# Turning probabilities on TensorE for two more steps, moving row sums, router roots and one key load in a fused attention and mixture kernel

## The reference

```
k_p, v_p = k.reshape(B,H,72,8,64).mean(3), v.reshape(B,H,72,8,64).mean(3)
attn = softmax(q @ k_p.T / sqrt(64));  x = (attn @ v_p) as 4608 x 512
h = x @ w_in;  g = max(h,0) + alpha*min(h,0);  x = g @ w_out          # 512 -> 2048 -> 512
logits = (x/|x|) @ (emb/|emb|).T / tau;  e = argmax;  gate = softmax(logits)[e]
out[token] = gate * (max(x[token] @ w1[e], 0) @ w2[e])                # 512 -> 1024 -> 512
```

## Time and profile before

| what | value |
|---|---|
| median of the runs | 1460.33 us |
| profiled execution, own time | 1461.15 us |
| its span | 1458.8 us |
| PE busy | 1403.1 us (96%) |
| DVE / ACT / POOL busy | 54% / 48% / 47% |
| mean granted clock of TensorE | 0.986 |

### The profile page before, as it was taken

One profiled execution on the slowest core, in us unless ns is written; L12 is line 12 of the kernel. 1 busy time (PEld: TensorE's weight loads), 2 busy tenths in 40 slices (PEclk: granted clock), 3 DMA queues, 4 the chain that ended last, 5 costly groups with the idle time before them and its releaser, 6 DMA issues.

```text
span 1458.8 us, 21254 instructions
## 1 busy us (share of the span) xinstructions
PE 1403.1 (96%) x7245; PEld 1152.0 (79%) x7245; DVE 792.8 (54%) x1498; ACT 693.1 (48%) x1022; POOL 687.7 (47%) x613
## 2 busy tenths in 40 slices
PE   8999989989989989989999999999999999999997
PEld 7887877868868767868788788888888878887876
DVE  7665766666757757757657576690002710066560
ACT  5434533433443443442433322544667666666664
POOL 4542243253243343342232233366666866577773
PEclk9999999999999999999999999999999999999999
DMA  8535242251352242332232220344433964369551
GB/s 249 173 108 153 67 120 67 60 125 56 75 119 60 68 114 59 82 91 70 47 87 52 59 87 22 135 167 130 96 88 80 219 185 98 79 145 238 143 113 26
DMA packets 204614, 153.57 MB, mean 105 GB/s; under 512 B 147036, under 2 KB 163420, under 8 KB 204384
## 3 DMA queue, kind: packets, MB, share of 16 engines
q1 hardware_dynamic: 59200, 99.20, 21.7%
q10 hardware_dynamic: 137280, 34.10, 14.4%
q0 software_dynamic: 8032, 18.93, 4.0%
HBM read 92.34 MB, written 29.43 MB: 83 GB/s over the span
## 4 chain that ended last, share of the span: by engine, by line
PE 72%; DMA 9%; DVE 6%; POOL 4%; issue 4%; ACT 3%; SPq 1%; ACTq 1%; DVEq 0%; POOLq 0%
PE y_ps L869 19%; PE h_ps L853 18%; PE y_ps L1010 14%; PE y_ps L976 14%; PE h_ps L813 2%; DMA shared<-in_k 2%; PE step_ps L769 2%; DMA x_dram<-shared 2%; DMA shared<-shared 2%; PE h_ps L988 1%; DMA shared<-in_v 1%; DVE weight_parts L1298 1%; POOL shared L1840 1%; DVE junk L1184 1%; POOL g_lo L1851 1%
## 5 line engine op out<-in xcount | busy, mean ns | idle before, releaser
L1851 POOL TENSOR_TENSOR g_lo<-g_full,g_hi 128x512 fp32r<-128x512 f32 x144 | 192.8, 1339 | 541.7 <-ACT g_hi L1536 541.7
L853 PE MATMUL h_ps<-x_hi_in,weight_parts 128*128 128x512 f32 x1144 | 373.5, 390 | 0.0
L869 PE MATMUL y_ps<-weight_parts,g_hi 128*128 128x512 f32 x1152 | 368.1, 401 | 2.1 <-POOL g_lo L1851 2.1
L869 PEld LDWEIGHTS y_ps<-weight_parts,g_hi 128*128 128x128 f32 x1152 | 218.4, 193 | 49.6 <-issue 2.4
L853 PEld LDWEIGHTS h_ps<-x_hi_in,weight_parts 128*128 128x128 f32 x1144 | 214.9, 188 | 44.6
L976 PE MATMUL y_ps<-weight_parts,x_hi_in 128*128 (+1 forms) x1032 | 242.0, 390 | 1.9 <-DVE weight_parts L1298 1.9
L869 PE MATMUL y_ps<-weight_parts,g_lo 128*128 128x512 f32 x576 | 228.5, 397 | 0.0
L976 PEld LDWEIGHTS y_ps<-weight_parts,x_hi_in 128*128 128x128 f32 x1032 | 193.3, 188 | 42.6 <-issue 2.7
L853 PE MATMUL h_ps<-x_lo_in,weight_parts 128*128 128x512 f32 x572 | 222.6, 389 | 0.0
L1165 DVE TENSOR_SCALAR g_full<-h_ps,alpha 128x512 f32<-128x512 f32 x144 | 107.7, 748 | 209.6 <-PE h_ps L853 207.4
L1536 ACT ACTIVATE g_hi<-g_full 128x512 fp32r<-128x512 f32 x144 | 90.7, 630 | 253.2 <-PE y_ps L869 171.0
(11 more groups left out here) (233 smaller groups left out, 1799.4 us busy)
## 6 DMA issues: line engine op xcount, KB each, us to landing
shared<-in_w SPq DMA_DIRECT2D x8, 2048.0 KB, 9.6
emb_all<-in_w SPq DMA_DIRECT2D x8, 2048.0 KB, 9.4
y_dram<-y_rows SPq DMA_DIRECT2D x9, 1024.0 KB, 4.4
shared<-in_q SPq DMA_DIRECT2D x34, 256.0 KB, 2.9
shared<-in_v SPq DMA_DIRECT2D x29, 288.0 KB
x_dram<-shared SPq DMA_DIRECT2D x32, 256.0 KB, 3.3
y_rows<-x_dram SPq DMA_DIRECT2D x32, 256.0 KB, 3.5
shared<-in_k SPq DMA_DIRECT2D x26, 288.0 KB, 3.7
```

Source lines behind the costliest of these rows:

```text
L853: mm = pe.matmul(h_ps[:, f % 2, :], w[:, k, f * P:(f + 1) * P], x[:, k, :], start=(n == 0), stop=(n == 3 * DC - 1))
L869: mm = pe.matmul(y_ps[:, j, :], a[:, f % 2, j * P:(j + 1) * P], w[:, f, :], start=(f == 0 and n == 0), stop=(f == FC - 1 and n == 2))
L1851: pool.tensor_tensor(gl[:, f % 2, :], g_full[:, f % 2, :], gh[:, f % 2, :].bitcast(F32), ALU.subtract).then_inc(gl_done, 1)
```

## The change

It has five parts. `TURN` becomes 10, so that steps 8 and 9 are turned by PE and the DMA turns from step 10 on. From step 10 on `row_scale` moves from the chunk behind the scores into the scores' own chunk (behind the first of the three dots, at chunk 12 behind `router_logits`), and `norm` with it, ahead of that chunk's `g_lo` on POOL. ACT's `root` moves from chunk 11 to chunk 9. SP issues the keys of chunk 12 ahead of the next tile's x, and DVE pools the keys of chunk 13 behind `router_choose` and `router_gate`.

```diff
-TURN = 2 * FIRST
+TURN = 2 * FIRST + QBUFS
@@ sync, tile
                         store_x(s)
+                        if 1 <= i <= BATCH - 3 and f in (6, 9, 12):
+                            load_k(PAIRS * (i + 2) + (f - 6) // 3)
                         if s == last_step(i + 1):
                             load_x(i + 1)
...
-                    elif i <= BATCH - 3:
-                        if f in (6, 9, 12):
-                            load_k(PAIRS * (i + 2) + (f - 6) // 3)
-                        elif f == FC - 1:
-                            sp.wait_ge(plane_joined, 2 * (last_step(i + 1) + 2 - TURN))
-                            load_k(PAIRS * (i + 2) + PAIRS - 1)
+                    elif i <= BATCH - 3 and f == FC - 1:
+                        sp.wait_ge(plane_joined, 2 * (last_step(i + 1) + 2 - TURN))
+                        load_k(PAIRS * (i + 2) + PAIRS - 1)
@@ vector, tile
                     s = sum_step(i, f)
-                    if s is not None:
+                    if s is not None and s < TURN:
                         row_scale(s)
...
-                        dots(i - 1, 3 * (f - 1), min(3 * f, DOTS))
+                        n = 3 * (f - 1)
+                        dots(i - 1, n, n + 1)
+                        if s is not None and s >= TURN:
+                            row_scale(s)
+                        dots(i - 1, n + 1, min(n + 3, DOTS))
...
-                    if n is not None:
+                    if n is not None and (i == 0 or f < 13):
                         sum_keys(n)
...
                         router_logits(i - 1)
+                        if s is not None and s >= TURN:
+                            row_scale(s)
                     if i and f == 13:
                         router_choose(i - 1)
                         router_gate(i - 1)
+                        if k_at(i, f) is not None:
+                            sum_keys(k_at(i, f))
@@ scalar, tile: root
-                    if i and f == 11:
+                    if i and f == 9:
@@ gpsimd, tile
                     s = sum_step(i, f)
-                    if s is not None:
+                    if s is not None and s < TURN:
+                        norm(s)
+                    s = score_step(i, f)
+                    if s is not None and s >= TURN:
                         norm(s)
```

## The result

The changed kernel took 1429.31 us (median of 4 runs, 1427.89 to 1430.99) against 1462.88 us of the kernel before on the same chip (4 runs): ratio 0.9772, 95% interval 0.9744 to 0.9800. Forecast were 1421 us and a range of 1413 to 1434. The direction and the main mechanism held; the gain was 33.6 us and not 39.5, and what is missing comes from waits at the ends of tiles, which I had priced at 1.0 us and which cost 9.5.

The account below looks back on a forecast made before the run. PE was taken to bound the kernel, leaving idle and low-clock time to win. Terms -22.1 - 9.4 - 7.9 - 1.4 - 1.6 + 1.9 + 1.0 = -39.5 gave 1421 us, range 1413 to 1434.

Parts of the forecast that it names:

- What bounds the kernel: Whole kernel: PE, busy 1403.1 of 1458.8 us; to win are 55.7 us of idle time and the low-clock time.
- Part 1: Chunk 13, tiles 1 to 5: keys asked earlier, pooled behind the choice; `ranks` waits go, -22.1 us, low clock behind, -9.4.
- Part 2: Chunks 6, 9, 12: sums and scaling one chunk up, roots at chunk 9; `values` waits -7.9 us, low clock at 621.6 -1.4.
- the floor of 1.5 us: Joins at chunks 6 and 9: 0.1 to 0.2 us of wait left at each of 10 places, 1.5 us of 9.4.
- The rule of the Trainium skill: DVE and POOL share an exclusive port pair: `norm` waiting for one dot cuts the 2.0 us gain to 1.4, two dots 0.8.
- Part 3: Steps 8 and 9 turned by PE: +1.9 us of turns, -1.6 us as the wait at tile 0's end goes.
- Part 4: Ends of tiles 1 to 5, without the turning pause: slow planes make `g_lo` of chunk 15 late, +1.0 us taken.
- A plane's way took up to 5.4 us: Ends of tiles 1 to 5: time from a plane's issue to the next copy, at most 5.4 us, used to time `g_lo`.
- the upper bound that I had given: Ends of tiles 1 to 5: with the slowest planes seen, 1.9 us late in each of five, 9.5 us.
- The rival of the tile ends: Tile ends: slow planes make a new wait, 3.9 us plus 1.9 of low clock in five tiles; 1449 us, chance 0.07.
- One of my own signs of being wrong: PE waiting for `g_lo` or next x at tile ends, or for joins at chunks 6, 9, 12 by over 0.5 us each.

Follow-up runs that it names:

- the two halves: Kernel before with one key edit each: keys of chunk 13 only pooled behind choice and gate, 1437.7 us; keys only asked for ahead of x, 1431.5 us.
- the turn back at step 8: Changed kernel with the DMA turning steps 8 and 9 again, sums and scaling still moved from step 10 on: 1427.7 us, ratio 0.9745.
- sums late: Changed kernel with row sums and scaling one chunk behind the scores again; keys, roots and turn as changed: 1433.0 us, ratio 0.9776.
- the root at 11: Changed kernel with the router's roots back at chunk 11, all else kept: 1425.1 us, ratio 0.9752.
- small x: Changed kernel with the x loads of tiles 2 to 6 fetching only 32 of 512 columns of each piece: 1415.8 us (one run).
- half of x later: Changed kernel with the third and fourth x piece of tiles 2 to 6 asked for behind the values' load of chunk 12: 1415.9 us, ratio 0.9649.
- after: The changed kernel itself, with all five parts, in its first profile, against the kernel before: 1429.31 us, ratio 0.9772.
- the keys alone asked ahead: Kernel before with one edit, SP asking for the keys ahead of x, DVE still pooling them ahead of the choice: 1431.5 us, ratio 0.9784.
- the change again: Changed kernel run once more, unaltered, on the same chip as later follow-ups: 1426.0 us, ratio 0.9762 to the kernel before.
- the values held: Changed kernel with the load of chunk 13's values held back at the ends of tiles 1 to 5 until x's last piece landed: 1437.1 us, ratio 0.9825.
- their pooling behind `g_lo`: Changed kernel with POOL's pooling of chunk 13's values moved behind `g_lo` of chunk 14: 1430.5 us, ratio 0.9762.

## Why the prediction was right, and where its size was off

**What bounds the kernel.** Right: each wait removed for good was won, and with the `ranks` waits the low clock behind them.

**Part 1 (-22.1 and -9.4).** Right, both. No `ranks` wait and no low clock at this place is left. I had counted the two halves as one edit; each alone does it. The low clock was counted too low: I had followed it for twelve matmuls, but it lasted longer. In the 6 us behind the waits of tiles 1 to 5 the clock of before was 0.65, 0.53, 0.74, 0.62 and 0.72, which loses 6 x 1.74 = 10.4 us, as in tile 2:

```profile
324.51:330.51 6.00, 6.00 (x20) 4.76 (x21) 3.52 (x15) 1.64 (x2) 0.39 (x1) 0.53 0.64 96
```

**Part 2 (-7.9 and -1.4).** Right as a step: all 9.4 us at `values` went, and the floor of 1.5 us that I had left at chunks 6 and 9 is not there. The root's move is worth the 6.2 us at chunk 12 and the sums' move the 3.1 us at chunks 6 and 9. The 6 us behind the wait of 621.64 ran at 0.72, so they lost 1.7 us and not 1.4. The rule of the Trainium skill (SBUF — State Buffer, Who interferes with whom) that spoke against the move was seen, and no wait at `values` came of it. A dot took a mean of 757 ns before and takes 849 now, and `norm` went from 1150 to 1361 ns, while the sums' second instruction went from 698 to 214:

```profile
L1183 DVE CUSTOM_DVE_ANT_0 junk<-y_rows,emb_all 128x512 bf16<-128x512 f32 x256 | 206.2, 849 | 0.3 <-issue 0.3
...
L1847 POOL TENSOR_TENSOR shared<-shared,row_scale 128x576 f32<-128x576 f32 x35 | 47.7, 1361 | 153.5 <-DVE row_scale L1142 153.5
```

These rows agree with the rule as I used it for the dots: in tile 2 a dot that began at 288.55, beside `norm` (288.09 to 289.63), took 1.63 us. The sums' second instruction reads a single tensor, so the two inputs that I named can't be what held it.

**Part 3 (+1.9 and -1.6).** Right within the noise: the whole 1.8 us at tile 0 went, and with the turn back at step 8 the time is the same.

**Part 4 (+1.0) is the step that was mis-sized.** "A plane's way took up to 5.4 us" was read from planes that left 3.7 us or more behind x. My working had the plane leave at 212.4, 3.0 us behind x, and kept that duration. It left only 0.7 us behind x in all five tiles and took 8.3 to 9.0 us. In tiles 2 to 5 the store's landing released it, the same that x waits for, as here in tile 2, where x was issued at 308.78:

```profile
308.77 0.69 ACT L1506 ACTIVATE shared<-shared 128x576 uint16<-128x576 uint16 x1 [2.02 <-DMA x_dram<-shared]
```

Even at the place that I had given it, planes took up to 7.3 us (sums late). And I had no term for the values of chunk 13, for which POOL stood 7.29 us in tile 1. The wait that followed was for `g_lo` of chunk 14, not of chunk 15 as I had followed it.

Measured: the `g_lo` line rose from 2.1 to 7.8 us, though the 1.8 us at tile 0 had gone. So the ends of tiles 1 to 5 cost 2.68 + 1.62 + 1.45 + 0.42 + 1.38 = 7.55 us of standing and, in tile 1 alone, 7.36 - 5.44 (two layers of 2.72) = 1.9 us of low clock: 9.5 us where I had 1.0. That this equals the upper bound that I had given is chance: that bound was five waits of 1.9 us for `g_lo` of chunk 15, with no low clock. The rival of the tile ends was right in kind and too high in price, since the low clock followed one wait out of five. One of my own signs of being wrong, a wait for `g_lo` at tile ends, did show.

**The sum with the measured terms.** -22.1 - 10.4 - 9.4 - 1.7 - 1.8 + 1.9 + 9.5 = -34.0, and the dense stage won 33.9. So the forecast missed part 4 by 8.5 us, and other terms that I had set too low (low clock, values, tile 0) gave 3.0 back. That the time still lay in the range owes something to this.

**Where the gain of part 2 went.** The root's move wins 6.2 us at chunk 12, and the tiles' ends take them back, as the run with the root at 11 shows by its equal time. The small x (1415.8 us) shows that x's transfer is the price, and half of x later (1415.9 us) shows that most of it can be had. Two engines stand at a tile's end. When the plane leaves early, POOL stands for the values (after); when it leaves late, ACT comes late to `g_hi` (sums late). Still open: why a plane that leaves 3.3 us behind x took 7.3 us with the sums late, while one 4.5 us behind took 3.5 us with the keys alone asked ahead; and in which part of the chip plane and x meet, for which no run was made.

## What to carry to other kernels

A duration of a transfer read from a trace belongs to the moment in which it ran: when an edit moves a transfer, look what is in flight at the new place, and price it with that company. Issuing it earlier can leave its end where it was. When two engines wait for two colliding transfers, reordering one engine's work only shows the other; split or delay the transfer that nobody needs soon. And a wait removed early in a repeated block counts only once the block's end has been followed to the next engine that stands.

## What the runs showed of the hardware

- A DMA transpose within SBUF (a plane) was back in 3.2 to 4.9 us when the x issued 0.7 us ahead of it was small, and took 6.2 to 10.6 us when that x was four loads of 256 KB (planes 0.7 us behind x in the change, the change again, the roots at 11, the values held and their pooling behind `g_lo`). Left 3.7 us or more behind x it took 3.3 to 5.8 us. At the ends of tiles 1 to 5 the median landing of a piece of x was 3.4 to 3.7 us before and 6.0 to 6.4 us in the changed kernel.
- With half of x later the plane's way ranged from 3.9 to 8.2 us and the landing of a piece from 3.8 to 6.1.
- The clock did not follow every short stop. Behind waits of 1.62, 1.45, 0.42 and 1.38 us the next two layers took 5.74 to 5.87 us, behind 2.68 us 7.36. With the values held back, stops of 3.35, 4.28, 2.27, 3.17 and 3.16 us in tiles 1 to 5 were followed by 8.59, 7.89, 5.73, 7.37 and 5.75 us: two stops of the same length, and only one with a low clock behind it. A shorter stop can have one too: with the roots at 11 PE stood 0.82 us ahead of the `values` at 303.83 and then ran the small matmuls of `values` and `scores`, and the layer 2 at 305.97 took 4.53 us.
